# Attention with plain fp32 matmuls, and inputs handed over transposed and tiled

## The reference

```python
# 1. attention: B=2, H=8, S=768, D=64; key j is kept for query i if j < 8 or 0 <= i-j < 96
scores = q @ k.T / 8 - slope[h] * dist          # dist = i-j in the band, 96 for the 8 global keys
a = exp(scores - max); a = a / (sum(a) + 1e-9)
x = (a @ v), heads side by side                 # (2, 768, 512)
# 2. rotation and mixing of tokens
theta = x @ w_theta
y = w_tok_r @ (x * cos(theta)) + w_tok_i @ (x * sin(theta))      # over the 768 tokens
u = x + y
v2 = u + relu(u @ w_ch)
# 3. gated convolution
h = relu(v2 @ w_in)                             # 512 -> 1024
out = (h * sigmoid(conv3(h, conv_w))) @ w_out
```

## Time and profile before

| | us |
|---|---|
| median of 3 runs | 521.23 |
| lowest, highest run | 520.74, 523.04 |
| span of the profiled execution, first to last instruction | 518.9 |
| what the median has beyond that span | 2.3 |
| PE busy | 441.9 (85%) |
| DVE busy | 310.1 (60%) |
| ACT busy | 230.2 (44%) |
| POOL busy | 153.1 (30%) |

### The profile page before, as it was taken

How to read it: one execution, slowest core, us unless ns; L and a number is a source line. 1 busy time by engine, 2 the same in 40 slices (tenths; PEclk the granted TensorE clock), 3 DMA queues, 4 the chain that set the end, 5 groups by cost and what they waited for, 6 DMA issues and landing times.

```text
span 518.9 us, 8296 instructions
## 1 busy us (share of the span) xinstructions
PE 441.9 (85%) x3224; PEld 379.4 (73%) x3224; DVE 310.1 (60%) x671; ACT 230.2 (44%) x429; POOL 153.1 (30%) x101
## 2 busy tenths in 40 slices
PE   2658888888697666989999999788898899997997
PEld 1547777777475455778788887778898788996886
DVE  5798888888549999911221202877856750167620
ACT  3446777777337657600100101443465541455521
POOL 4271122222407766830000000444403350023340
PEclk9978999999979988999999999988999899998999
DMA  6861666512500100010130001121000002100012
GB/s 134 204 143 29 125 124 122 114 46 42 197 2 0 61 0 1 0 63 0 62 141 2 0 1 66 55 76 46 1 1 0 0 1 81 42 0 1 1 39 83
DMA packets 48600, 27.37 MB, mean 53 GB/s; under 512 B 41840, under 2 KB 42160, under 8 KB 48560
## 3 DMA queue, kind: packets, MB, share of 16 engines
q1 hardware_dynamic: 48560, 26.83, 20.1%
HBM read 20.46 MB, written 3.15 MB: 45 GB/s over the span
## 4 chain that ended last, share of the span: by engine, by line
PE 52%; DVE 31%; issue 9%; ACT 6%; DMA 1%; POOL 0%; DVEq 0%; SPq 0%; ACTq 0%
PE bank L449 28%; PE bank L663 13%; PE bank L510 6%; DVE gf L1195 3%; DVE zf L1124 3%; DVE vtmp L1169 2%; DVE th_r L1112 2%; DVE bias L985 2%; DVE x L963 2%; DVE sc L934 2%; PE bank L461 2%; ACT h_sb L849 2%; DVE kT L917 2%; ACT cv L854 1%; DVE cv L1185 1%
## 5 line engine op out<-in xcount | busy, mean ns | idle before, releaser
L449 PE MATMUL bank<-z,wT 128*128 128x512 f32 x432 | 101.1, 392 | 2.4 <-DVE wT L1087 2.4
L449 PEld LDWEIGHTS bank<-z,wT 128*128 128x128 f32 x432 | 80.3, 188 | 19.2 <-DVE wT L1087 2.9
L449 PE MATMUL bank<-vT,win 128*128 128x384 f32 x384 | 71.2, 346 | 9.7 <-ACT h_sb L849 7.9
L449 PEld LDWEIGHTS bank<-vT,win 128*128 128x128 f32 x384 | 69.5, 196 | 11.4 <-ACT h_sb L849 9.2
L663 PE MATMUL bank<-wout,g 128*128 128x512 f32 x288 | 65.7, 389 | 0.0
L663 PEld LDWEIGHTS bank<-wout,g 128*128 128x128 f32 x288 | 54.0, 188 | 11.1
L437 POOL TENSOR_TENSOR g<-gf,g 128x768 fp32r<-128x768 f32 x16 | 34.4, 2154 | 91.4 <-ACT g L868 91.4
L449 PE MATMUL bank<-wth,xT 128*128 128x512 f32 x144 | 42.9, 455 | 16.1 <-DVE xT L1095 16.1
L1142 DVE TENSOR_TENSOR x<-bank,x 128x512 f32<-128x512 f32 x12 | 8.3, 690 | 78.4 <-PE bank L449 78.4
L449 PEld LDWEIGHTS bank<-wth,xT 128*128 128x128 f32 x144 | 30.7, 221 | 25.5 <-DVE xT L1095 18.9
L1185 DVE SCALAR_TENSOR_TENSOR cv<-h_sb,convw,cv 128x768 f32<-128x768 f32 x16 | 16.3, 1018 | 54.1 <-ACT cv L854 54.1
(11 more groups left out here) (101 smaller groups left out, 754.7 us busy)
## 6 DMA issues: line engine op xcount, KB each, us to landing
qkraw<-q_in SPq DMA_DIRECT2D x16, 192.0 KB, 3.7
qkraw<-k_in SPq DMA_DIRECT2D x16, 192.0 KB, 4.2
vraw<-v_in SPq DMA_DIRECT2D x16, 192.0 KB, 4.3
out<-ob SPq DMA_DIRECT2D x12, 256.0 KB, 2.0
vold<-vown SPq DMA_DIRECT2D x8, 361.9 KB
wrows<-w_tok_r_in SPq DMA_DIRECT2D x6, 384.0 KB, 3.0
wrows<-w_tok_i_in SPq DMA_DIRECT2D x6, 384.0 KB, 3.6
winraw<-w_in_in SPq DMA_DIRECT2D x4, 512.0 KB, 4.5
```

Of the source, the lines that this page charges most:

```text
L449: last = pe.matmul(dst, w[a], m[b], start=(i == 0 and j == 0), stop=(i == n - 1 and j == 2))
```

## The change

The host hands over, beside q, k and v as they are, three laid-out arrays. `qk_laid[p]` has for each pair of heads the transposed q and the transposed k with the 8 global columns ahead of each tile (128 by 1584 fp32, 792 KB a pair); `v_laid[p]` has values, a column of ones, and the older and global keys' values in place (780 KB a pair); `w_tok[m]` has the transposed blocks of both token matrices (768 KB for each m). One DMA loads each. Of the attention's work, `transpose_qk`, `high_qk`, `low_qk`, `high_v`, `mid_v`, the POOL splits of v, the DMAs of L280 and L281, `low_p` and the scaling go. Scores and values are single fp32 matmuls. The output of `weighted_v` has two banks, bank 7 and bank 0. The token matrices are split without a transpose, 1536 columns at a time, with m = 0 on POOL ahead of theta.

```diff
-                for j, (a, b) in enumerate(((0, 0), (0, 1), (1, 0))):
-                    for h in range(2):
-                        rows = slice(h * D, (h + 1) * D)
-                        last = pe.matmul(S_BANK[u % 2][h][:, BAND - (c1 - c0):BAND], qT[rows, pp, a, i * P:(i + 1) * P],
-                                         kT[rows, pp, b, c0:c1], start=(j == 0), stop=(j == 2))
+                for h in range(2):
+                    rows = slice(h * D, (h + 1) * D)
+                    pe.matmul(S_BANK[u % 2][h][:, BAND - (c1 - c0):BAND], qk_sb[rows, pp, i * P:(i + 1) * P],
+                              qk_sb[rows, pp, S + c0:S + c1], start=True, stop=True).then_inc(scores_ready, 1)
...
-                if u >= 1:
-                    pe.wait_ge(x_done, u)
+                if u >= 2:
+                    pe.wait_ge(x_done, u - 1)
...
-                        for part in range(2):
-                            for first, width in ((0, D + 1), (D + 1, D), (2 * D + 1, D)):
-                                last = pe.matmul(O_BANK[:, h * OW:h * OW + width], ...
+                        last = pe.matmul(O_BANK[u % 2][:, h * OW:(h + 1) * OW], pT[:, u % 2, slot * P:(slot + 1) * P],
+                                         v_sb[:, pp, i, chunk, h, :], start=(chunk == 0), stop=(chunk == chunks - 1))
...
-                act.activation(d, src, ACT.Copy, scale=P_SCALE).then_inc(p_hi, 1)
+                act.activation(d, src, ACT.Copy).then_inc(pt_copied, 1)
...
+            def load_qk(p):
                 if p >= 2:
-                    sp.wait_ge(qk_transposed, 3 * (p - 1))
+                    sp.wait_ge(scores_ready, 2 * NT * (p - 1))
+                sp.dma_start(qk_sb[:, p % 2, :], qk_laid[p]).then_inc(qk_in[p % 2], 16)
+            def load_v(p):
+                if p >= 2:
+                    sp.wait_ge(o_ready, NT * (p - 1))
+                sp.dma_start(v_sb[:, p % 2], v_laid[p]).then_inc(v_in[p % 2], 16)
...
             load_qk(0)
+            load_v(0)
+            load_qk(1)
+            load_v(1)
+            sp.dma_start(wraw[:], w_theta.rearrange("(c p) n -> p c n", p=P)).then_inc(wraw_in, 16)
+            load_w_tok(0)
+            load_w_tok(1)
...
+            pool.wait_ge(wrows_in[0], 16)
+            low = split_weight(wrows[:, 0], (wT[0][:, 0], wT[0][:, 1]), w0_ready, wth_step)
...
+            def high_rows(m):
+                if m == 1:
                     act.wait_ge(r_ready, TT)
                     act.wait_ge(trig_ready, TT)
+                else:
                     act.wait_ge(y_ready, MIXES.index((m - 2, B - 1)) + 1)
+                act.wait_ge(wrows_in[m % 2], 16 * (m // 2 + 1))
+                act.activation(wT[m % 2][:, 0], wrows[:, m % 2], ACT.Copy).then_inc(w_hi, 1)
...
+            def low_rows(m):
+                dve.wait_ge(w_hi, m)
+                dve.tensor_tensor(wT[m % 2][:, 1], wrows[:, m % 2], wT[m % 2][:, 0].bitcast(F32), ALU.subtract)\
+                   .then_inc(w_lo, 1)
...
-        ROWS_AT_MIX = {1: [(1, 2)], 3: [(2, 0), (2, 1)], 4: [(2, 2), (3, 0)], ...
+        W_AT_MIX = {3: 2, 4: 3, 6: 4, 8: 5}
```

More of the change, by code:

```diff
@@ L35, with build @@
 PI_BELOW = 3.1415925
-def build(nc, q, k, v, n_global, n_local, w_theta, w_tok_r, w_tok_i, w_ch, w_in, conv_w, w_out, out):
+def build(nc, q, k, v, qk_laid, v_laid, n_global, n_local, w_theta, w_tok, w_ch, w_in, conv_w, w_out, out):
     B, H, S, D = q.shape
@@ L185, in build @@
         block = ctx.enter_context(nc.Block())
-        QT_BANK = bank[0]
         S_BANK = [[bank[1], bank[2]], [bank[3], bank[4]]]
         PT_BANK = [bank[5], bank[6]]
-        O_BANK = bank[7]
+        O_BANK = [bank[7], bank[0]]
         def pair(p):
             return p // HP, 2 * (p % HP)
[L196 to L216, removed]
         def choose(eng, banded, general):
@@ L264, in banded @@
-            def banded():
[L265 to L294, removed]
@@ L451, in product @@
                     last.then_inc(ready, 1)
-            def transpose_qk(p, group):
-                pp = p % 2
-                if group == 0:
-                    pe.wait_ge(qk_in[pp], 16 * 4 * (p // 2 + 1))
-                if p >= 1:
-                    pe.wait_ge(qk_lo, 3 * p + group)
-                for slot in range(4):
-                    which, tile = divmod(4 * group + slot, NT)
-                    last = pe.transpose(qk_group_bank(p, group)[:, slot * P:(slot + 1) * P], qkraw[:, pp, which, tile, :], ident[:])
-                last.then_inc(qk_transposed, 1)
             def scores(u):
@@ L557, in _, with tokens_split @@
             choose(pe, banded, general)
[L559 removed]
+            Y_BANK = [bank[6], bank[7]]
             U_BANK, R_BANK = [bank[0], bank[1]], [bank[2], bank[3]]
[L562 to L572 removed]
+            def tokens_split(m):
+                if m == 0:
+                    pe.wait_ge(w0_ready, 1)
+                else:
+                    pe.wait_ge(w_lo, m)
             def transpose_u(c, blk):
@@ L670, in _ @@
         def _(act):
-            def high_qk(p, group):
-                n = 3 * p + group
-                act.wait_ge(qk_transposed, n + 1)
-                if group == 0 and p >= 2:
-                    act.wait_ge(scores_ready, 2 * NT * (p - 1))
-                pp = p % 2
-                for slot, cnt, which, tile in GROUPS[group]:
-                    last = act.activation(qk_place(pp, 0, which, tile, cnt), qk_bank(p, group, slot, cnt, which), ACT.Copy)
-                if group == 1:
-                    last = act.activation(kt_global(pp, 0), kt_global_bank(p), ACT.Copy)
-                last.then_inc(qk_hi, 1)
             def exps(u):
@@ L990, in banded @@
                 make_bias(1)
-                for group in range(3):
-                    low_qk(0, group)
                 maxima(0, 0)
```

235 lines of the change are left out of this document (69 added, 166 removed).

## The result

The changed kernel takes 556.19 us (median of 4 runs, 555.33 to 556.79) against 521.17 for the kernel before on the same chip. The ratio is 1.0663, with an interval of 1.0626 to 1.070. It is slower by 35 us; the forecast was 27.7 us faster. The profiled execution has a span of 554.0 us.

A forecast was written before the change was run, and what follows sets the result against it. The attention was taken as bound by DVE's loop, then by a 2.10 us ACT and PE loop. Gains 23.5 + 1.8 - 4.8 + 7.0 = 27.5 us gave 493.5 us, range 484 to 519.

The forecast's parts named there:

- The price of a plain fp32 matmul: Attention on PE: a unit's transposes, scores and values take 1.7 us, bounds 0.70 and 3.76.
- rival 3: Attention: granted clock falls to 1.2 GHz, loop 2.54 us, a pair 14.4, total 514 us; chance 0.08.
- must be within 2.10 us: Attention: PE's work per unit must fit under the 2.10 us loop through ACT and PE, or PE becomes the bound.
- Rival 2: Attention: slower, as plain fp32 matmuls pay passes with loads that don't overlap; 531 us, 565 at upper bound 3.76; chance 0.13.
- Twice a transpose's price: Attention: scores and values priced at twice a plain fp32 transpose, making PE's unit 2.10 us with the transposes.
- The estimate from the four passes: Attention: four array passes per fp32 product; scores 0.41 to 0.82, values 0.62, PE's unit 1.47 to 1.88 us.
- Steady part: Attention: pairs shrink from 13.9 to 11.9 us, eight times, gaining 16 us.
- Start: Attention's beginning: first maxima earlier because DVE's subtraction of q and k low parts goes; gain 3.0 us, bounds 0 and 3.5.
- End of the attention: Attention in all 23.5 us shorter, including 4.5 at its head and tail; the stall at w_theta's split stays.
- Theta and on to product 1: Theta gains 1.8 us on DVE; then product 1 waits 3.3 longer and starts slowly for 1.5, a 4.8 loss.
- Mixing: Mixing on PE: token transposes and waits for their splits go, gaining 7.0 us of 98.3.
- Rival 4: Attention: loads bind, a pair's two loads taking 13.9 us, steady gain gone, total 509 us; chance 0.04.

The follow-up runs named there:

- e5: Changed kernel with 16 bf16 matmuls before the first scores, 10 after the second, and POOL's w_theta split held until all biases are built; 491.23 us.
- e1: Changed kernel with three added bf16 matmuls of 382 columns in every attention unit, results never read; 507.18 us.
- e2: Changed kernel with 16 bf16 matmuls of 512 columns before the first scores and 10 after the second, none later; 559.55 us.
- e6: Changed kernel with one added bf16 matmul of 382 columns in every attention unit, nothing at the start; 497.68 us.
- e11: Changed kernel with scores and values each as three fp32r products, plus one added bf16 matmul of 380 columns per unit; 607.11 us.
- e12: Changed kernel with w_theta's split held back and 384-column bf16 matmuls in PE's waits at the start, before theta and in mixing; 483.21 us.
- e9: Changed kernel with POOL's w_theta split held until all biases are built, no added matmuls; 557.81 us.

## Why the prediction was wrong

**The step that failed** is "The price of a plain fp32 matmul" together with the dismissal of rival 3. Every price in it, and the test "must be within 2.10 us", was for 2.4 GHz, and the full clock was taken as given from the 0.99 in the earlier trace rows. That 0.99 belonged to a PE that ran 24 f16 matmuls per unit, which the change takes away. The kernel before fell to 1.2 GHz in its attention too (1.10 in the earlier trace rows) and recovered by its own work (a rise at 33.3, and 0.63 for the same four at 33.93); the changed one has nothing that does this. At 1.2 GHz the unit is 0.85 + 1.08 + 1.90 = 3.83 on PE and PE becomes the bound.

**Rival 3 named the cause and had the wrong size and too small a chance, 0.08.** It doubled the transposes and left scores and values as they were, and so came to 514. With the forecast's own 1.7 doubled, PE's unit is 3.4, and 8 x 5 x (3.4 - 2.1) = 52 us on 493.5 make 545.5, near the 556 measured. The reason against it, gaps on PE "much as they will be", looked at the gaps and not at the kind of work between them. Its test failed as well: it asked for a granted clock under 0.9, and the column says 1.00, for want of an entry before 188.1. What told the level was the duration of an operation that the change left alone, the transposes of p, and where the first entry stands.

**Rival 2 came near for another reason.** Its upper bound of 3.76 us a unit gave 565, and the unit measured is 3.83. But it meant loads that don't overlap, at full clock; e5 has 0.44 to 0.66 + 0.59 + 1.04 for the same work.

**The price at full clock** was on the right side. e5's transposes at their own 0.44, scores of 0.59 and values of 1.04 make 2.07, against 1.7 taken and 2.10 as the limit; e1 has 0.44 + 0.59 + 0.84 = 1.87. "Twice a transpose's price", which the text gave as 2.10, was the better reading. The estimate from the four passes of the Trainium skill ("FP8 and Floating Point Precision", TensorE Precision Notes) was 1.47 to 1.88; scores at 0.59 lie in its 0.41 to 0.82, values at 0.84 to 1.04 above its 0.62.

**Term by term, with the clock held (e5).**
- Steady part: pairs of 12.3 for 11.9 forecast. PE's 2.07 leaves it beside the ACT and PE loop, and now one, now the other ends last. The mechanism was right; the term gives 8 x (13.9 - 12.3) = 13 for 16.
- Start: the first maxima came at 11.46 in the kernel after, 6.4 earlier than the 17.90 of the earlier trace rows, for 3.0 forecast. The load landed before 7.09, and the bias began at 10.43 for 12.42: DVE's first cast took 2.18 us in the kernel before and 0.17 now, which the forecast did not foresee. In the kernel before it ended at 6.20, as POOL's filling of `vold` did (2.86 to 6.17), and the change drops that filling; that the cast waited for it is likely and not tested. (In e5 they come at 12.61, behind the added matmuls.)
- End of the attention: forecast 142.4 - 23.5 = 118.9, measured 115.99 in e5. It includes the stall at w_theta's split, which the forecast left in place and which e5 takes away.
- Theta and on to product 1: forecast 1.8 shorter and 4.8 longer, of which 1.5 as a slow start inside mixing, so 1.5 longer to product 1; measured 0.9 longer. ACT took 1.47 (1.5 forecast) and DVE 2.73 (3.1).
- Mixing: 7.0 shorter forecast, 5.1 measured with the slow start in it. Seven products at 8.18 are 57.3, and 59.00 is 1.7 more (1.5 forecast), so the term itself is 6.8.
- Rival 4, loads that bind: `qk_laid` lands in 4.3 us at the median and PE has no wait for it in the steady part. It fell.

With the clock held, the terms came out within 3.4 us of what was forecast, with errors both ways. That e5 lies at 491.2 where 493.5 was forecast is in part luck: e5 is not the change as it was forecast but has the stall taken away, and its attention ends 2.9 early while the rest is 1.2 longer.

**What stays open.** Which part of the attention's work counts for nothing towards a rise, the fp32 transposes, the plain products or both, was not separated. The Trainium skill ("TensorE: Matmul & The Clock Gate", Part 4, PE-mode transpose) says that transposes don't count as PE-busy in the same way for the clock. In e2 the granted clock is 0.50 in the windows 24 to 60 and 120 to 180 us, with PE busy throughout; that agrees, but the work there holds plain products too, of which the page says nothing. Open is also why one added matmul sufficed in e6 and not in e11, where the unit was longer and held fp32r products of 66 columns. And no run adds matmuls to the kernel before, which also falls to 1.2 GHz at times, so how much of e12's lead over it belongs to the change, and how much to the clock alone, is not known.

## What to carry to other kernels

Price a change of PE's data type at both clock levels, and ask whether the work left on PE can bring the clock up; if the answer isn't in a trace, the lower level is a rival with the whole of PE's work doubled. Read the level from the duration of an operation that the change did not touch, not from the clock column alone. Where the work holds the clock but does not raise it, as here, a few bf16 matmuls in gaps in which PE waits anyway can decide whether a change pays: with one POOL split put off, they took this kernel from 556 to 483 us.

## What the runs showed of the hardware

- Plain fp32 products and fp32 transposes kept PE busy for 146.00 of 146.00 us without leaving 1.2 GHz, and held 2.4 GHz for 100 us once it was there (e5, whose four transposes take 0.44 to 0.66).
- A plain fp32 matmul leaves two weight loads and two matmuls in the record. At 2.4 GHz a unit's two of 232 columns, one on each half of the rows, took 0.59 us together and one of 65 columns 0.21 to 0.26; at 1.2 GHz 1.08 and 0.475.
- The clock column showed 1.00 through attentions that ran at 1.2 GHz from their first transposes, because the record's first entry is the first rise (188.1 us in the kernel after, 188.3 in e9), and 0.50 where the level had fallen on the way (e2).
- Two DVE bias instructions with both tensors in SBUF take 0.59 us together (e5, 19.90); beside POOL's cast and its subtraction of 4.54 us the same two took 6.40 (e2).
